# The second layer's activation: VectorE's clip and rest take the products from PSUM, not from ScalarE's copy

## The chip, the cores and the metric

One core of one Trainium2 chip (trn2). The metric is the device time of one execution of the whole program, in microseconds (us). The kernel before was run three times; one more execution was recorded by the hardware profiler.

## What is computed

Attention with a learned position bias, then two feed-forward layers, all in fp32 on 2304 tokens of 512 features:

```
x = attention(q, k, v, bias)                         # 4 x 8 heads, 576 x 64
x = max(max(x @ w1, x @ w2), x @ w3) @ w_out         # first layer, 768 hidden
h = x @ w_in                                         # second layer, 2304 x 2048
g = where(h >= 1, h, where(h <= -1, 0, (h + 1)**2 / 4))
out = g @ w_out                                      # 2304 x 512
```

The change is in the second layer. There the kernel uses that g is the square of 0.5 * clip(h, -1, 1) + 0.5, plus max(h - 1, 0), which the code calls clip (`tb`) and rest (`tc`).

## The kernel before

Weights, tokens and activations are each split into a high and a low fp32r part, and every product is three passes of TensorE (high times high, high times low, low times high).

The second layer runs last. Its work is ND = 72 items: 9 blocks of 256 tokens (b), with 8 items (j) in each, and n = 8b + j. An item holds two tiles of 128 hidden features, so 512 columns, one PSUM bank. For each n TensorE does in this order: `d_products(n)` (L1320), 24 matmuls into the item's bank; then `d_sums(n - 2)` (L1339), 21 matmuls that multiply the activation of the item two before with w_out. These are the seven products of a Strassen scheme, in seven banks. The seven sums run on over the 8 items of a block. `n_bank(n)` (L304) gives the bank of an item: 0, 1 and 2 for the first three, and bank 0 for all later ones, because banks 1 to 7 then hold the sums. So `d_products(n)` for n >= 3 waits until bank 0 has been read (L1324), and the very first `d_sums` waits until all of the first three banks have been read (L1348), since it writes banks 1 and 2.

The activation of item n goes back and forth between ScalarE and VectorE:

- ScalarE, L862: copies the bank (128x512) to `ta` in SBUF and counts `d_cp`. It waits for the products (`d_in`), and for the rest of the item before, as `ta` is single.
- VectorE, L1089: clip of `ta` into `tb`; L1090: rest of `ta` into `tc`. It waits for `d_cp` and for its own `g_lo` of the item before (`d_g_ok`).
- ScalarE, L866: square of `tb`, in place. VectorE, L1095: adds `tc`. VectorE, L1097 to L1102: four small sums for the Strassen scheme.
- ScalarE, L875 and L877: `g_hi`, in two parts. VectorE, L1104 and L1107: `g_lo`, in two parts, with `d_g_ok` at the end. `d_sums(n)` waits for that.

Each engine works through its own list in order, and some items have more in the list. In item j = 1 of every block but the first, behind the rest, `sums_first` of the block before (L844 on ScalarE, L1059 to L1064 on VectorE) takes sums from PSUM as TensorE ends them, and behind `g_lo` comes `sums_rest` (L849, L851; L1071 to L1077). Behind `g_lo` of j = 6, and in front of the clip of j = 7, VectorE does two each of `low_xd` (L1041), the low part of the next block's tokens; ScalarE does their high part (L831) in j = 5 and in front of j = 7. SyncE loads the weights of w_in in a ring of four; each load waits for `d_in` (L491).

Of the kernel before, what the change touches and what calls it, by code (L numbers as in the profile page):

```python
# [7 lines left out]
ALU = mybir.AluOpType  # L8
ACT = mybir.ActivationFunctionType
# [6 lines left out]
def build(nc, q, k, v, w1, b1, w2, moe_w1, moe_w2, moe_w3, moe_w_out, moe2_w_in, moe2_w_out, out):  # L16
# [55 lines left out]
    def sb(name, shape, dt=F32, c=None):  # L72
        return (c or ctx).enter_context(nc.sbuf_tensor(name, shape, dt))

    def sem(name):
        return ctx.enter_context(nc.semaphore(name))

    with ctx:
# [40 lines left out]
        with moe:  # L119
# [3 lines left out]
            ta = sb("ta", [P, 2 * SBT], c=moe)  # L123
            tb = sb("tb", [P, 2 * SBT], c=moe)
            tc = sb("tc", [P, 2 * SBT], c=moe)
# [17 lines left out]
        ps = ctx.enter_context(nc.psum_tensor("ps", [P, 8, 512], F32))  # L143
# [50 lines left out]
        win_in = [sem(f"win_in{r}") for r in range(WRING)]  # L194
        wt_in = [sem(f"wt_in{j}") for j in range(NPAIR)]
        d_x_hi, d_x_ok, d_x_used = sem("d_x_hi"), sem("d_x_ok"), sem("d_x_used")
        d_in, d_cp, d_clip, d_rest, d_sq, d_g = (sem(n) for n in
                                                 ("d_in", "d_cp", "d_clip", "d_rest", "d_sq", "d_g"))
        d_s13, d_s2, d_s4 = sem("d_s13"), sem("d_s2"), sem("d_s4")
        d_g_hi, d_g_ok = sem("d_g_hi"), sem("d_g_ok")  # L200
        d_item, d_acc, d_acc_cp, d_post = sem("d_item"), sem("d_acc"), sem("d_acc_cp"), sem("d_post")
# [89 lines left out]
        def ring_at(k):  # L291
            return k % WRING * WIN
# [8 lines left out]
        def x_slot(b, kt):  # L301
            return (KT * b + kt) % XRING

        def n_bank(n):  # L304

            return n if n < 3 else 0
# [355 lines left out]
        def _(act):  # L662
# [164 lines left out]
            def high_xd(b, kt):  # L827

                if b and kt >= XRING - KT:
                    act.wait_ge(d_x_used, (KT - 2) * (b - 1) + kt - 1)  # L830
                act.activation(xd_hi[:, x_slot(b, kt), :], xT[:, kt, x_cols(b)], ACT.Copy).then_inc(d_x_hi, 1)  # L831
# [7 lines left out]
            def sums_first(b):  # L839

                act.wait_ge(d_acc, 6 * b + 1)
                if b:
                    act.wait_ge(d_post, 7 * b)
                act.activation(u_sb, ps[:, P1_BANK, 0:HD], ACT.Copy).then_inc(d_acc_cp, 1)  # L844
# [9 lines left out]
            for n in range(ND):  # L854
                b, j = n // NPAIR, n % NPAIR
                if j == NPAIR - 1 and b + 1 < NSB:
                    high_xd(b + 1, 2)
                    high_xd(b + 1, 3)
                act.wait_ge(d_in, 2 * n + 2)
                if n:  # L860
                    act.wait_ge(d_rest, n)
                act.activation(ta[:, :], ps[:, n_bank(n), :], ACT.Copy).then_inc(d_cp, 1)  # L862
                if j == 1 and b:
                    sums_first(b - 1)
                act.wait_ge(d_clip, n + 1)
                act.activation(tb[:, :], tb[:, :], ACT.Square, scale=0.5, bias=0.5).then_inc(d_sq, 1)  # L866
                if j == 1 and b:
                    sums_rest(b - 1)
                if j == NPAIR - 3 and b + 1 < NSB:
                    high_xd(b + 1, 0)  # L870
                    high_xd(b + 1, 1)
                act.wait_ge(d_g, n + 1)
                if n >= 2:
                    act.wait_ge(d_item, n - 1)
                act.activation(g_hi[:, n % 2, 0:GA], tb[:, P:4 * P], ACT.Copy).then_inc(d_g_hi, 1)  # L875
                act.wait_ge(d_s4, n + 1)
                act.activation(g_hi[:, n % 2, GA:GS].rearrange("p (s c) -> p s c", s=4), s_sub,  # L877
                               ACT.Copy).then_inc(d_g_hi, 1)
# [4 lines left out]
        def _(dve):  # L883
# [197 lines left out]
            for n in range(ND):  # L1081
                b, j = n // NPAIR, n % NPAIR
                if j == NPAIR - 1 and b + 1 < NSB:
                    low_xd(b + 1, 2)
                    low_xd(b + 1, 3)
                dve.wait_ge(d_cp, n + 1)
                if n:
                    dve.wait_ge(d_g_ok, n)
                dve.tensor_scalar(tb[:, :], ta[:, :], -1.0, 1.0, ALU.max, ALU.min).then_inc(d_clip, 1)  # L1089
                dve.tensor_scalar(tc[:, :], ta[:, :], -1.0, 0.0, ALU.add, ALU.max).then_inc(d_rest, 1)  # L1090
                if j == 1 and b:
                    sums_first(b - 1)
                dve.wait_ge(d_rest, n + 1)
                dve.wait_ge(d_sq, n + 1)
                dve.tensor_tensor(tb[:, :], tb[:, :], tc[:, :], ALU.add).then_inc(d_g, 1)  # L1095
                dve.wait_ge(d_g, n + 1)
                dve.tensor_tensor(s1, a21, a22, ALU.add).then_inc(d_s13, 1)  # L1097
                dve.tensor_tensor(s3, a11, a21, ALU.subtract).then_inc(d_s13, 1)
                dve.wait_ge(d_s13, 2 * n + 2)
                dve.tensor_tensor(s2, s1, a11, ALU.subtract).then_inc(d_s2, 1)  # L1100
                dve.wait_ge(d_s2, n + 1)
                dve.tensor_tensor(s4, a12, s2, ALU.subtract).then_inc(d_s4, 1)  # L1102
                dve.wait_ge(d_g_hi, 2 * n + 1)
                dve.tensor_tensor(g_lo[:, n % 2, 0:GA], tb[:, P:4 * P], g_hi[:, n % 2, 0:GA].bitcast(F32), ALU.subtract)  # L1104
                dve.wait_ge(d_s4, n + 1)
                dve.wait_ge(d_g_hi, 2 * n + 2)
                dve.tensor_tensor(g_lo[:, n % 2, GA:GS].rearrange("p (s c) -> p s c", s=4), s_sub,  # L1107
                                  g_hi[:, n % 2, GA:GS].rearrange("p (s c) -> p s c", s=4).bitcast(F32),
                                  ALU.subtract).then_inc(d_g_ok, 1)
                if j == 1 and b:  # L1110
                    sums_rest(b - 1)
                if j == NPAIR - 2 and b + 1 < NSB:
                    low_xd(b + 1, 0)
                    low_xd(b + 1, 1)
# [4 lines left out]
        def _(pe):  # L1119
# [200 lines left out]
            def d_products(n):  # L1320

                b, j = n // NPAIR, n % NPAIR
                if n >= 3:
                    pe.wait_ge(d_cp, n)  # L1324
                for f in range(2):
                    k = 2 * n + f
                    pe.wait_ge(win_in[k % WRING], 16 * (k // WRING + 1))
                    for kt in range(KT):
                        if j == 0 and f == 0:
                            pe.wait_ge(d_x_ok, KT * b + kt + 1)  # L1330
                        at, s = ring_at(k) + kt * P, x_slot(b, kt)
                        for i, (lo, x) in enumerate(((0, xd_hi), (0, xd_lo), (KT * P, xd_hi))):
                            last = pe.matmul(ps[:, n_bank(n), f * SBT:(f + 1) * SBT], w_all[:, at + lo:at + lo + P],  # L1333
                                             x[:, s, :], start=(kt == 0 and i == 0), stop=(kt == KT - 1 and i == 2))
                        if j == NPAIR - 1 and f == 1 and kt < KT - 2:
                            last.then_inc(d_x_used, 1)
                    last.then_inc(d_in, 1)

            def d_sums(n):  # L1339

                b, j = n // NPAIR, n % NPAIR
                pe.wait_ge(d_g_ok, n + 1)
                if n == 0:
                    pe.wait_ge(c_y_ok, KT * NBLK)
                if b == 0:
                    pe.wait_ge(wt_in[j], 64 if j in PIECES else 16)
                if n == 0:
                    pe.wait_ge(d_cp, 3)  # L1348
                for i, (bank, g, w) in enumerate(PRODUCTS):
                    if j == 0 and b:  # L1350
                        if bank == P1_BANK:
                            pe.wait_ge(d_acc_cp, 3 * (b - 1) + 1)
                        elif i < 4:
                            pe.wait_ge(d_post, 7 * (b - 1) + i)
                        else:
                            pe.wait_ge(d_acc_cp, 3 * (b - 1) + min(i - 2, 3))
                    at = wt_at(j) + w * HD
                    for m, (x, lo) in enumerate(((g_hi, 0), (g_hi, TCOLS), (g_lo, 0))):
                        last = pe.matmul(ps[:, bank, 0:HD], x[:, n % 2, g * P:(g + 1) * P],  # L1359
                                         w_all[:, at + lo:at + lo + HD], start=(j == 0 and m == 0),  # L1360
                                         stop=(j == NPAIR - 1 and m == 2))
                    if j == NPAIR - 1 and i < 6:
                        last.then_inc(d_acc, 1)
                last.then_inc(d_item, 1)
# [31 lines left out]
```

## Time and profile before

| | us |
|---|---|
| median of 3 runs | 1020.13 |
| lowest and highest | 1017.62, 1020.18 |
| the profiled execution, its time | 1020.09 |
| its span in the trace | 1018.3 |
| TensorE busy | 991.1 (97% of the span) |
| VectorE busy | 616.4 (61%) |
| ScalarE busy | 509.4 (50%) |
| GpSimd busy | 347.4 (34%) |

The second layer starts at about 619 us of the span and goes to its end. Between the span and the time of the profiled execution lie 1.8 us that the trace does not show. In the trace PE is TensorE's matmuls, DVE is VectorE, ACT is ScalarE, and PEclk the clock that TensorE was granted, as a share of full speed. Matmuls overlap: one of 256 columns has a length of 0.28 us in the trace, and the next starts 0.12 us after it.

### The profile page before, as it was taken

Reading aid. Unit: us, or ns where it says so; the run is one execution under the profiler, and the core shown is the slowest. Engines: PE = TensorE matmul, PEld = TensorE weight load, DVE = VectorE, ACT = ScalarE, POOL = GpSimd, SP = SyncE. Lnnn points to the kernel's source line nnn. Section 1 sums busy time; section 2 is a strip of 40 time slices with the busy share of each in tenths; the row PEclk is TensorE's granted clock in tenths of the full one; section 3 lists DMA queues with packets and bytes.
Section 4 is the critical chain, followed back from the end, with each engine's and each line's share of the span. In section 5 each row is a group of like instructions: output and inputs, shape, how many; then the busy total and the mean of one; then the engine's idle time right before and its main releaser. Section 6 shows DMA issues by size and latency. Waiting matters only on the chain.

```text
span 1018.3 us, 23175 instructions
## 1 busy us (share of the span) xinstructions
PE 991.1 (97%) x8832; PEld 897.6 (88%) x8832; DVE 616.4 (61%) x1509; ACT 509.4 (50%) x1034; POOL 347.4 (34%) x522
## 2 busy tenths in 40 slices
PE   6979999999999999999999998999999999999998
PEld 3567777777767999999999998999999999999998
DVE  8957667666683242324231315677777877778776
ACT  8968778788793321212121213444554554545443
POOL 1059888888874878677300000000000000000000
PEclk9979999999999999999999999999999999999999
DMA  5982534425312464665510067866657667666772
GB/s 130 268 240 55 161 72 119 109 53 154 95 34 75 133 223 170 230 235 209 222 84 0 9 223 309 271 215 205 212 190 220 199 215 210 204 211 188 226 219 72
DMA packets 122149, 169.71 MB, mean 167 GB/s; under 512 B 67008, under 2 KB 84416, under 8 KB 120256
## 3 DMA queue, kind: packets, MB, share of 16 engines
q1 hardware_dynamic: 121952, 168.37, 53.0%
q8 instruction: 63, 1.03, 0.4%
q14 instruction: 38, 0.31, 0.1%
q10 hardware_dynamic: 96, 0.00, 0.0%
HBM read 129.64 MB, written 38.70 MB: 165 GB/s over the span
## 4 chain that ended last, share of the span: by engine, by line
PE 72%; DVE 2%; ACT 1%; issue 0%; DVEq 0%; ACTq 0%
PE ps L1265 22%; PE ps L1333 20%; PE ps L1359 18%; PE ps L1292 7%; PE ps L1216 2%; PE ps L1156 2%; PE ps L1177 1%; PE ps L1191 0%; DVE x_lo L979 0%; DVE tb L1095 0%; PE ps L1130 0%; ACT tb L866 0%; ACT ta L862 0%; DVE s_sb L926 0%; DVE g_lo L1107 0%
## 5 line engine op out<-in xcount | busy, mean ns | idle before, releaser
L1265 PE MATMUL ps<-x_hi,w_all 128*128 128x384 f32 x864 | 227.2, 336 | 3.0 <-DVE x_lo L979 1.8
L1333 PE MATMUL ps<-x_hi,w_all 128*128 128x256 f32 x1152 | 219.3, 283 | 1.2 <-DMA w_all<-win_scratch 1.2
L1359 PE MATMUL ps<-w_all,g_hi 128*128 128x256 f32 x1008 | 185.9, 284 | 2.6 <-ACT ta L862 2.4
L1333 PEld LDWEIGHTS ps<-x_hi,w_all 128*128 128x128 f32 x1152 | 184.8, 192 | 1.6 <-DMA w_all<-win_scratch 1.6
L1333 PE MATMUL ps<-x_lo,w_all 128*128 128x256 f32 x576 | 163.0, 283 | 0.0
L1265 PEld LDWEIGHTS ps<-x_hi,w_all 128*128 128x128 f32 x864 | 157.5, 189 | 5.3 <-DVE x_lo L979 2.3
L1359 PEld LDWEIGHTS ps<-w_all,g_hi 128*128 128x128 f32 x1008 | 158.3, 193 | 3.0 <-issue 2.6
L926 DVE CUSTOM_DVE_ANT_0 s_sb<-ps,bias_h 128x576 f32<-128x576 f32 (+1 forms) x160 | 114.8, 754 | 71.5 <-PE ps L1156 53.7
L1265 PE MATMUL ps<-x_lo,w_all 128*128 128x384 f32 x432 | 145.1, 336 | 0.0
L1359 PE MATMUL ps<-w_all,g_lo 128*128 128x256 f32 x504 | 143.1, 284 | 0.0
L586 POOL TENSOR_SCALAR probs<-probs,row_inv 128x576 f32<-128x576 f32 (+1 forms) x160 | 120.8, 766 | 18.7 <-DVE row_inv L956 18.1
L714 ACT ACTIVATE probs<-s_sb,row_min 128x576 f32<-128x576 f32 (+1 forms) x160 | 122.2, 769 | 1.8 <-DVE row_min L926 1.7
L1333 PEld LDWEIGHTS ps<-x_lo,w_all 128*128 128x128 f32 x576 | 110.6, 192 | 0.0
L1359 PEld LDWEIGHTS ps<-w_all,g_lo 128*128 128x128 f32 x504 | 97.4, 193 | 0.0
L1014 DVE TENSOR_TENSOR tb<-ps,ta 128x384 f32<-128x384 f32 x36 | 20.0, 557 | 121.9 <-PE ps L1265 121.3
L812 ACT ACTIVATE g_hi<-tc 128x384 fp32r<-128x384 f32 x36 | 18.9, 524 | 125.7 <-DVE tc L1021 125.7
L1265 PEld LDWEIGHTS ps<-x_lo,w_all 128*128 128x128 f32 x432 | 81.6, 189 | 0.0
L1292 PE MATMUL ps<-g_hi,w_all 128*128 128x384 f32 x288 | 78.7, 334 | 0.0
L1216 PE MATMUL ps<-p_t,v_in 128*64 128x320 f32 (+1 forms) x512 | 76.0, 418 | 0.0
L726 ACT ACTIVATE p_t<-ps 128x512 f32<-128x512 f32 x80 | 47.8, 597 | 49.3 <-PE ps L1177 48.4
L1156 PEld LDWEIGHTS ps<-qk_hi 64*128 64x128 f32 x320 | 36.7, 189 | 39.1 <-DVE row_min L926 22.6
L866 ACT ACTIVATE tb<-tb 128x512 f32<-128x512 f32 x72 | 45.6, 633 | 47.9 <-DVE tb L1089 47.9
(115 smaller groups left out, 1806.5 us busy)
## 6 DMA issues: line engine op xcount, KB each, us to landing
w_all<-win_scratch SPq DMA_DIRECT2D x144, 512.0 KB, 4.3
wt_scratch<-w_all SPq DMA_DIRECT2D x8, 1792.0 KB, 6.8
w_all<-wt_scratch SPq DMA_DIRECT2D x6, 1792.0 KB, 7.5
bias_scratch<-p_t SPq DMA_DIRECT2D x36, 296.0 KB, 4.6
win_scratch<-w_all SPq DMA_DIRECT2D x8, 1024.0 KB, 7.0
raw<-in_moe_w_out SPq DMA_DIRECT2D x22, 256.0 KB, 7.1
bias_h<-bias_scratch SPq DMA_DIRECT2D x16, 288.0 KB, 4.2
raw<-in_moe_w SPq DMA_DIRECT2D x18, 256.0 KB, 3.0
```

What stands on the lines that cost most here:

```text
L586: pool.tensor_scalar(pr, pr, row_inv[0:n, r, h:h + 1], 1.0, ALU.mult, ALU.mult).then_inc(p_norm, 1)
L714: act.activation(probs[0:n, r, h * S:(h + 1) * S], s_sb[0:n, (2 * u + h) % 4, :], ACT.Exp, scale=-1.0, bias=row_min[0:n, r, h:h + 1], accu ...
L726: act.activation(p_t[:, i % 2, :, :, t * P:t * P + HALF].rearrange("p h c j -> p (h c) j"), ps[:, X_BANK, :].rearrange("p (c j) -> p c j", ...
L866: act.activation(tb[:, :], tb[:, :], ACT.Square, scale=0.5, bias=0.5).then_inc(d_sq, 1)
L926: dve.tensor_tensor_reduce(s_sb[0:n, (2 * u + h) % 4, :].rearrange("p (c x) -> p c x", c=2), ps[0:n, 2 * h:2 * h + 2, 0:HC], bias_h[0:n, h ...
L1014: dve.tensor_tensor(tb[:, 0:BLK], ps[:, H_BANK_C[1], 0:BLK], ta[:, 0:BLK], ALU.max).then_inc(c_m1, 1)
L1156: return pe.matmul(ps[:, 2 * h + c, 0:HC], a[HALVES[h], i % 2, 0, t * P:(t + 1) * P], b[HALVES[h], i % 2, 1, c * HC:(c + 1) * HC], start=( ...
L1216: last = pe.matmul(ps[h * HALF:(h + 1) * HALF, O_BANK_A, 0:cols.stop - cols.start], v_in[:, i % 2, h, kt, :], tqk[:, i % 2, 0, cols] if kt ...
L1265: last = pe.matmul(ps[:, bank, 0:BLK], w[:, at:at + P], x[:, kt, :], start=(kt == 0 and n == 0), stop=(kt == KT - 1 and n == 2))
L1292: last = pe.matmul(ps[:, Y_BANK + dt, 0:BLK], w[:, at:at + P], g[:, ft % 2, :], start=(opens and i == 0), stop=(closes and i == 2))
L1333: last = pe.matmul(ps[:, n_bank(n), f * SBT:(f + 1) * SBT], w_all[:, at + lo:at + lo + P], x[:, s, :], start=(kt == 0 and i == 0), stop=(k ...
L1359: last = pe.matmul(ps[:, bank, 0:HD], x[:, n % 2, g * P:(g + 1) * P], w_all[:, at + lo:at + lo + HD], start=(j == 0 and m == 0), stop=(j = ...
```

## The change

```
@@ act, for n in range(ND)
-                act.wait_ge(d_in, 2 * n + 2)
-                if n:
-                    act.wait_ge(d_rest, n)
-                act.activation(ta[:, :], ps[:, n_bank(n), :], ACT.Copy).then_inc(d_cp, 1)
@@ dve, for n in range(ND)
-                dve.wait_ge(d_cp, n + 1)
+                dve.wait_ge(d_in, 2 * n + 2)
                 if n:
                     dve.wait_ge(d_g_ok, n)
-                dve.tensor_scalar(tb[:, :], ta[:, :], -1.0, 1.0, ALU.max, ALU.min).then_inc(d_clip, 1)
-                dve.tensor_scalar(tc[:, :], ta[:, :], -1.0, 0.0, ALU.add, ALU.max).then_inc(d_rest, 1)
+                dve.tensor_scalar(tb[:, :], ps[:, n_bank(n), :], -1.0, 1.0, ALU.max, ALU.min).then_inc(d_clip, 1)
+                dve.tensor_scalar(tc[:, :], ps[:, n_bank(n), :], -1.0, 0.0, ALU.add, ALU.max).then_inc(d_rest, 1)
@@ pe, d_products(n)
                 if n >= 3:
-                    pe.wait_ge(d_cp, n)
+                    pe.wait_ge(d_rest, n)
@@ pe, d_sums(n)
                 if n == 0:
-                    pe.wait_ge(d_cp, 3)
+                    pe.wait_ge(d_rest, 3)
```

The semaphore `d_cp` is gone. Nothing else changes; `ta` stays in use in the first layer.

## Rows read from the trace of the kernel before

**Rows 1.** The page's first part: busy us, share of span, instructions of each engine.

```profile
PE 991.1 (97%) x8832; PEld 897.6 (88%) x8832; DVE 616.4 (61%) x1509; ACT 509.4 (50%) x1034; POOL 347.4 (34%) x522
```

**Rows 2.** Busy time by stretch, 40 us of the second layer (stretch, length, engines, clock).

```profile
740.00:780.00 40.00, 40.00 (x335) 40.00 (x335) 30.36 (x77) 19.72 (x35) 0.00 (x0) 1.00 0.65 203
```

**Rows 3.** Timeline of an ordinary item (j = 5), PE, ACT and DVE (start, length).

```profile
735.73 0.28 PE L1333 MATMUL ps<-x_hi,w_all 128*128 128x256 f32 x1
...
738.37 0.28 PE L1333 MATMUL ps<-x_hi,w_all 128*128 128x256 f32 x1
...
736.05 0.60 ACT L862 ACTIVATE ta<-ps 128x512 f32<-128x512 f32 x1 [1.03 <-PE ps L1333]
737.14 0.63 ACT L866 ACTIVATE tb<-tb 128x512 f32<-128x512 f32 x1 [0.49 <-DVE tb L1089]
...
736.68 0.43 DVE L1089 TENSOR_SCALAR tb<-ta 128x512 f32<-128x512 f32 x1 [0.87 <-ACT ta L862]
737.03 0.42 DVE L1090 TENSOR_SCALAR tc<-ta 128x512 f32<-128x512 f32 x1
737.88 0.69 DVE L1095 TENSOR_TENSOR tb<-tb,tc 128x512 f32<-128x512 f32 x1 [0.43 <-ACT tb L866]
```

**Rows 4.** Groups of VectorE by line and form (count, busy us, mean ns, idle before).

```profile
L940 DVE COPY p_t<-ps 128x512 f32<-128x512 f32 x64 | 43.8, 684 | 2.3 <-PE ps L1177 2.3
...
L1089 DVE TENSOR_SCALAR tb<-ta 128x512 f32<-128x512 f32 x72 | 30.6, 425 | 37.7 <-ACT ta L862 36.6
...
L915 DVE TENSOR_SCALAR p_t<-ps,nconst 128x592 f32<-128x592 f32 x1 | 0.8, 833 | 4.6 <-DMA bias_scratch<-p_t 4.6
```

**Rows 5.** Timeline of items j = 1 and 2 of block 1, DVE and PE.

```profile
671.88 0.43 DVE L1089 TENSOR_SCALAR tb<-ta 128x512 f32<-128x512 f32 x1 [0.87 <-ACT ta L862]
...
672.56 0.42 DVE L1059 TENSOR_TENSOR raw<-ps,raw 128x256 f32<-128x256 f32 x1
...
678.33 0.42 DVE L1089 TENSOR_SCALAR tb<-ta 128x512 f32<-128x512 f32 x1
...
678.97 0.28 PE L1333 MATMUL ps<-x_hi,w_all 128*128 128x256 f32 x1
```

**Rows 6.** Timeline where the first products of the layer pass on, ACT, DVE, PE.

```profile
622.12 0.60 ACT L862 ACTIVATE ta<-ps 128x512 f32<-128x512 f32 x1 [2.08 <-PE ps L1333]
...
631.12 0.58 ACT L862 ACTIVATE ta<-ps 128x512 f32<-128x512 f32 x1
...
622.85 0.43 DVE L1089 TENSOR_SCALAR tb<-ta 128x512 f32<-128x512 f32 x1 [2.66 <-ACT ta L862]
...
627.49 0.43 DVE L1089 TENSOR_SCALAR tb<-ta 128x512 f32<-128x512 f32 x1
...
631.85 0.77 PE L1359 MATMUL ps<-w_all,g_hi 128*128 128x256 f32 x2 [2.40 <-ACT ta L862]
```

**Rows 7.** Busy time by stretch, as rows 2: idle times of TensorE and its clock.

```profile
58.00:61.40 3.40, 1.38 (x6) 1.05 (x8) 2.18 (x5) 2.16 (x4) 0.00 (x0) 0.51 0.98 281
61.40:64.80 3.40, 3.33 (x19) 2.41 (x19) 1.52 (x5) 1.74 (x7) 2.51 (x6) 0.50 1.00 339
...
624.60:628.05 3.45, 2.28 (x17) 1.87 (x16) 2.94 (x9) 1.74 (x4) 0.00 (x0) 1.00 1.01 370
...
631.46:634.87 3.41, 3.02 (x14) 3.05 (x15) 2.79 (x7) 0.87 (x2) 0.00 (x0) 0.50 0.89 360
```

**Rows 8.** Timeline of the last two `d_sums`, PE.

```profile
1010.53 0.40 PE L1359 MATMUL ps<-w_all,g_hi 128*128 128x256 f32 x2
1010.77 0.28 PE L1359 MATMUL ps<-w_all,g_lo 128*128 128x256 f32 x1
1011.27 0.50 PE L1359 MATMUL ps<-w_all,g_hi 128*128 128x256 f32 x2 [0.21 <-DVE g_lo L1107]
```

**Rows 9.** Timeline of VectorE from item j = 6 to j = 7 of block 2.

```profile
745.92 0.69 DVE L1107 TENSOR_TENSOR g_lo<-raw,g_hi 128x512 fp32r<-128x512 f32 x1 [0.30 <-ACT g_hi L877]
746.53 1.43 DVE L1041 TENSOR_TENSOR x_lo<-xT,x_hi 128x256 fp32r<-128x256 f32 x4
747.87 0.42 DVE L1089 TENSOR_SCALAR tb<-ta 128x512 f32<-128x512 f32 x1
```

More of the change, by code:

```diff
@@ L196, in build @@
         d_x_hi, d_x_ok, d_x_used = sem("d_x_hi"), sem("d_x_ok"), sem("d_x_used")
-        d_in, d_cp, d_clip, d_rest, d_sq, d_g = (sem(n) for n in
-                                                 ("d_in", "d_cp", "d_clip", "d_rest", "d_sq", "d_g"))
+        d_in, d_clip, d_rest, d_sq, d_g = (sem(n) for n in ("d_in", "d_clip", "d_rest", "d_sq", "d_g"))
         d_s13, d_s2, d_s4 = sem("d_s13"), sem("d_s2"), sem("d_s4")
```

## The prediction

> **What bounds the kernel now.** I read the busy shares first: TensorE is busy for 97% of the span [rows 1]. Then the second layer by stretch: TensorE is busy for 40 of 40 us at full clock, VectorE for 30.4, ScalarE for 19.7 [rows 2]. So nothing that shortens an activation can help in the steady state. The change can only open gaps on TensorE, or close the two it has in this layer: 2.40 us before the first `d_sums` [rows 6] and 0.21 us before the last [rows 8]. I therefore read the timeline for slack. The question is how long after the end of an item's products its bank is released, and when TensorE wants it back.
>
> The products of an item end at 735.73 + 0.28 = 736.01, and TensorE starts the next products at 738.37, 2.36 us later [rows 3]. Before, the bank was free 0.64 us after the products' end (0.04 to the start of the copy, 0.60 for it). TensorE goes from item to item in 5.40 us (45 matmuls at 0.12 us; 746.53 - 735.73 is two of them).
>
> **Part 1: the copy goes from ScalarE.** That frees 0.60 us per item on an engine that is half idle [rows 2, 3]: worth nothing by itself, since TensorE covers it. What it gives is an earlier clip: before, 0.67 us after the products' end (736.68), now 0.04, as ScalarE's copy had it. That is 0.63 us.
>
> **Part 2: clip and rest read PSUM.** From SBUF one takes 0.425 us. The trace before has no such instruction on 128x512 of PSUM. The low end is 0.425, as from SBUF. The high end is 0.83: L915, the one tensor_scalar from PSUM, which is 592 wide and has an operand from memory more. I take 0.69, from the copy of exactly this shape out of PSUM (684 ns, 64 times) [rows 4]. That is 0.26 more than now, for each of two instructions. Two VectorE instructions overlap by 0.08 us (clip to rest 0.35 for 0.43) [rows 3]. So the rest starts 0.60 after the clip starts and ends 0.60 + 0.69 = 1.29 after it (before: 0.77). The square waits for the clip alone, so everything behind it starts 0.26 later counted from the clip; the longer rest ends beside the square, and the add (before: 1.20 after the clip; now 1.46) still finds it done. An item's chain on VectorE, clip to next clip with no idle time for its input, was 627.49 - 622.85 = 4.64 us [rows 6]; it becomes 4.90. That is below 5.40, so VectorE keeps up in ordinary items, with 0.50 to spare, and an ordinary item's `g_lo` comes 0.63 - 0.26 = 0.37 earlier. Its bank is free at 0.04 + 1.29 = 1.33 after the products' end, before 2.36. Cost: nothing; cover: 1.03 us.
>
> A table of the Trainium skill (VectorE: DVE Perf Modes, the section on the TRN2 errata) charges an fp32 single-source operation 58 cycles plus half the elements from SBUF and 120 cycles plus all of them from PSUM. At its 0.96 GHz the growth would be an estimated 0.33 us and not 0.26, and with the terms below the sum would come out about 2.5 us higher. The trace's SBUF row (0.425 against the table's 0.33) does not bear the table out, so I stay with the rows. The same page's advice, to copy PSUM to SBUF first if many operations follow, speaks against this change.
>
> **Part 3: the bank's release moves from ScalarE's copy to VectorE's queue.** This costs. The rest now stands behind everything that VectorE still has to do for the item before, and behind it wait TensorE's next products, then all after them. Three places have more in the queue.
>
> (a) Item j = 2 of blocks 1 to 8, eight times. Before, its clip started at 678.33, late because VectorE did `sums_first` and `sums_rest` first; TensorE's next products started at 678.97 [rows 5], covered since ScalarE had copied already. Now: the clip of j = 1 starts at 671.88 - 0.63 = 671.25; L1059 follows two instructions of 0.60 spacing later, at 672.45 (before 672.56, 0.68 behind the clip). From L1059 to the next clip took 678.33 - 672.56 = 5.77 us, mostly VectorE's own work, which stays. So the clip of j = 2 starts at 678.22, its rest ends at 679.51, and TensorE resumes some 0.10 later, at 679.61, in place of 678.97: 0.64 us. After a wait its first two matmuls take 0.50 and not 0.40 [rows 8], 0.10 more. 8 x 0.74 = 5.9 us. The next clip, at 678.22 + 4.90 = 683.12, is back inside the cover, as TensorE itself is now 0.74 later.
>
> (b) Item j = 7 of blocks 0 to 7, behind four `low_xd`. The clip started at 747.87 [rows 9] and comes 0.37 earlier, 747.50; the rest ends at 748.79, and 0.10 on, at 748.89, TensorE can go. It wants to at 746.81 + 2.36 = 749.17. Cost: nothing, with only 0.28 us of cover.
>
> (c) The start. The first `d_sums` waited until ScalarE's third copy ended (631.12 + 0.58 = 631.70) and started at 631.85 [rows 6]. ScalarE's third copy did not need VectorE's item 1 complete; VectorE's third rest does. The first clip can start at 622.12, the third two chains later, at 622.12 + 2 x 4.90 = 631.92, and its rest ends at 633.21. With the same 0.15 TensorE goes at 633.36: 1.5 us later.
>
> The idle time there grows from 2.4 to 3.9 us, and it has an effect on the clock. After the 2.40 us TensorE ran at half clock from 631.46 to 634.87 [rows 7], of which 3.0 us fell on work; that lost about half of it. If the clock comes back at the same moment as before, only 1.5 us of work is slow (0.8 us gained); if a further such stretch follows, 4.9 us is (0.9 lost). The stretch from 58.00 is nearest, where TensorE also had little to do at half clock and the next one stayed at half [rows 7]. I take +0.8 and keep both ends.
>
> **Part 4: the end.** The last `d_sums` waited for `g_lo`, at 1011.27, when it could have gone at 1010.77 + 0.12 = 1010.89 [rows 8]. `g_lo` comes 0.37 earlier, at 1010.90. Gain: 0.4 us.
>
> The weight loads of SyncE wait for `d_in`, which TensorE still gives: they move only with TensorE. GpSimd has no part.
>
> **Sum.** +1.5 (start) + 0.8 (clock) + 5.9 (eight waits) - 0.4 (end) = +7.8 us on the profiled execution's 1020.09 (span 1018.3, 1.8 around it), which is 0.04 below the median: **1027.9 us**.
>
> **Rivals.**
>
> *PSUM reads cost VectorE no more than SBUF's: not slower.* Then the rest ends 0.77 after the clip. In (a) L1059 would have to wait for ScalarE's and TensorE's first sums, the next clip starts near 677.9, the bank is free at 678.7, before 678.97: no wait. At the start the third rest ends at 622.12 + 2 x 4.64 + 0.77 = 632.17, 0.5 late; the clock gives or takes 0.8; the end gives 0.4. Sum: 1020 (1019.4 to 1021.0). It decides at a clip and rest below about 0.53 us each, as 0.64 us of wait holds each excess four times. For it: ScalarE reads PSUM as fast as SBUF (0.60 for the copy, 0.63 for the square [rows 3]). Against: the copy's 684 ns [rows 4]. 7%.
>
> *The reads cost 0.83 each.* Growth 0.40: the start is 4 x 0.14 = 0.6 later, each wait of (a) takes 4 x 0.14 = 0.56 more (8 x = 4.5), and (b) loses its cover: clip 0.14 later, rest's end 0.42 later in all, 0.14 beyond the 0.28 and 0.10 for the restart, 8 x 0.24 = 1.9. The end's gain goes down to 0.3. Sum 7.8 + 0.6 + 4.5 + 1.9 + 0.1: 1035. 7%.
>
> *The clock falls at the eight waits.* If each brings a stretch at half clock of 3.4 us, 1.7 are lost each time: 1027.9 + 13.6 = 1041.5. Against: two idle times of about 0.6 us near 625 to 628 us, with TensorE busy for 2.28 of 3.45, and the clock stayed at 1.00 [rows 7]. 3%.
>
> *The change does not do what it says*: not likely, the diff names every wait and both operands; no chance of its own.
>
> **How the numbers follow.** The forecast has 83%. Its own range: 1.5 us less if the clock returns early, 1 less if restarts are free (0.10 x 8, and 0.05 in the wake), 1.5 more if the reads take 0.73, 1 more if the clock stays down longer; and an execution can lie 2.5 us below the profiled one, as one of the three runs does. That gives about 1023.5 to 1030.5. Towards the dearer reads I extend it to 1032; the rivals at 1020, 1035 and 1041.5 lie outside, 17%. 0.3% is 3.1 us, about what a measurement of this kernel can tell from no change. Slower by more: the forecast but for a twentieth of it (the waits half as long), and both dearer rivals, 0.89. Within 0.3%: that twentieth and most of the first rival, 0.09. Faster: the first rival with the clock's gain in runs as low as the lowest, 0.02.
>
> **What would show it.** Clip and rest at 0.69 us each; the rest's end the releaser of L1333 eight times, in total some 5 us; the wait before the first L1359 3.9 us, with the row of the clock at half behind it; the wait before the last gone; L1089 without idle time at j = 7, and no wait of TensorE there; ScalarE 43 us less busy (72 x 0.60). I am wrong if TensorE has no idle time at j = 2, or has some in ordinary items, or if the reads take another time than the copy.

## The result, and the profile after

The changed kernel took 1027.37 us (median of 10 runs, 1023.11 to 1030.73), the kernel before 1019.19 us in the same ten rounds (1017.39 to 1021.82). The medians are 8.2 us apart. The ratio of the two, taken over all their runs, is 1.0077, with a 95% interval of 1.006 to 1.0095: 7.8 us slower (6.1 to 9.7). The recorded execution of the changed kernel took 1026.83 us, with a span of 1025.0.

The page's first part, and then the same 40 us by stretch as in [rows 2]:

```profile
PE 992.3 (97%) x8832; PEld 897.5 (88%) x8832; DVE 654.2 (64%) x1509; ACT 467.7 (46%) x962; POOL 346.8 (34%) x522
```

```profile
740.00:780.00 40.00, 39.56 (x329) 39.36 (x329) 34.35 (x78) 15.59 (x29) 0.00 (x0) 1.00 0.70 208
```

ScalarE lost 41.7 us of work and VectorE got 37.8 us more. TensorE, which was busy for 40 of 40 us before, now has a small gap in that stretch. What it waited for in the second layer, by the view of waits (in total, times, longest):

```profile
PE ps L1354 <- DVE tc L1085: 4.1, 1, 4.1
PE ps L1328 <- DVE tc L1085: 3.5, 8, 0.4
PE ps L1328 <- DMA w_all<-win_scratch: 1.1, 2, 0.6
```

The lines have moved by five: L1328 is `d_products`, L1354 `d_sums`, L1084 the clip, L1085 the rest. The first wait is the start (2.40 before), the eight are new, the third was there before (2 times, 1.2 us in total). The wait before the last `d_sums`, 0.21 us in [rows 8], is gone. The groups of VectorE, to set against [rows 4]:

```profile
L1084 DVE TENSOR_SCALAR tb<-ps 128x512 f32<-128x512 f32 x72 | 49.7, 690 | 22.3 <-PE ps L1328 20.3
L1085 DVE TENSOR_SCALAR tc<-ps 128x512 f32<-128x512 f32 x72 | 49.1, 681 | 0.0
```

Both take what the copy of that shape out of PSUM takes (684 ns), not the 425 of the read from SBUF. The timeline of the changed kernel: the start (against [rows 6]), items j = 1 and 2 of block 1 (against [rows 5]), j = 6 and 7 of block 2 (against [rows 9]), and the last instruction on VectorE:

```profile
617.52 0.28 PE L1328 MATMUL ps<-x_hi,w_all 128*128 128x256 f32 x1
...
632.01 0.76 PE L1354 MATMUL ps<-w_all,g_hi 128*128 128x256 f32 x2 [4.07 <-DVE tc L1085]
...
640.16 0.40 PE L1354 MATMUL ps<-w_all,g_hi 128*128 128x256 f32 x2
...
620.69 0.69 DVE L1084 TENSOR_SCALAR tb<-ps 128x512 f32<-128x512 f32 x1 [1.95 <-PE ps L1328]
...
625.67 0.69 DVE L1084 TENSOR_SCALAR tb<-ps 128x512 f32<-128x512 f32 x1
...
630.57 0.69 DVE L1084 TENSOR_SCALAR tb<-ps 128x512 f32<-128x512 f32 x1
631.18 0.68 DVE L1085 TENSOR_SCALAR tc<-ps 128x512 f32<-128x512 f32 x1
...
672.76 0.69 DVE L1084 TENSOR_SCALAR tb<-ps 128x512 f32<-128x512 f32 x1 [0.45 <-PE ps L1328]
673.37 0.68 DVE L1085 TENSOR_SCALAR tc<-ps 128x512 f32<-128x512 f32 x1
673.96 0.41 DVE L1054 TENSOR_TENSOR raw<-ps,raw 128x256 f32<-128x256 f32 x1
...
679.74 0.68 DVE L1084 TENSOR_SCALAR tb<-ps 128x512 f32<-128x512 f32 x1
680.34 0.68 DVE L1085 TENSOR_SCALAR tc<-ps 128x512 f32<-128x512 f32 x1
...
680.36 0.28 PE L1354 MATMUL ps<-w_all,g_lo 128*128 128x256 f32 x1
681.08 0.39 PE L1328 MATMUL ps<-x_hi,w_all 128*128 128x256 f32 x1 [0.44 <-DVE tc L1085]
...
749.07 1.43 DVE L1036 TENSOR_TENSOR x_lo<-xT,x_hi 128x256 fp32r<-128x256 f32 x4
750.41 0.68 DVE L1084 TENSOR_SCALAR tb<-ps 128x512 f32<-128x512 f32 x1
751.01 0.68 DVE L1085 TENSOR_SCALAR tc<-ps 128x512 f32<-128x512 f32 x1
...
752.08 0.28 PE L1328 MATMUL ps<-x_hi,w_all 128*128 128x256 f32 x1
...
1021.79 0.42 DVE L1072 TENSOR_TENSOR raw<-raw,acc_sb 128x256 f32<-128x256 f32 x1
```

How to read the eight waits: the rest of j = 2 ends at 680.34 + 0.68 = 681.02, and TensorE's products start at 681.08. With no wait they would have started at 680.36 + 0.12 = 680.48. That is 0.60 us, and 0.1 more for the restart. The record calls only 0.44 of it idle, since the last matmul is drawn 0.28 long. So a wait of x in the record costs x + 0.26.

The whole second layer can be cut into three parts by such rows: first products to first `d_sums`; from there to the second `d_sums`, in which the slow matmuls lie; and from there to the end of VectorE's last instruction. For the kernel before the rows are these, with 631.85 of [rows 6]:

```profile
618.97 0.28 PE L1333 MATMUL ps<-x_hi,w_all 128*128 128x256 f32 x1
...
638.65 0.40 PE L1359 MATMUL ps<-w_all,g_hi 128*128 128x256 f32 x2
...
1015.04 0.42 DVE L1077 TENSOR_TENSOR raw<-raw,acc_sb 128x256 f32<-128x256 f32 x1
```

Worked out so for every record but those with a moved wait, whose first `d_sums` is cut in two (us):

| kernel | to first sums | to second sums | the rest | layer |
|---|---|---|---|---|
| before | 12.88 | 6.80 | 376.81 | 396.49 |
| changed | 14.49 | 8.15 | 382.05 | 404.69 |
| start as before | 12.87 | 6.96 | 381.98 | 401.81 |
| changed at the start only | 14.48 | 6.95 | 376.80 | 398.23 |
| changed, late sums | 14.48 | 6.73 | 376.45 | 397.66 |
| release moved, no PSUM read | 14.05 | 6.95 | 378.97 | 399.97 |
| both mends | 12.89 | 6.95 | 376.45 | 396.29 |
| changed, two small reads more | 15.32 | 6.95 | 392.04 | 414.31 |
| changed, again a | 14.48 | 6.96 | 381.98 | 403.42 |
| changed, again b | 14.47 | 7.95 | 381.96 | 404.38 |
| changed, again c | 14.48 | 6.96 | 381.96 | 403.40 |

The layer of the changed kernel is 8.20 us longer: 1.61 at the start, 1.35 in slow matmuls, 5.24 in the rest (eight times 0.70, less 0.36 at the end). What comes before the layer was 1.45 us shorter in this record; it has no part in the change and differs from record to record. The first and third parts repeat within 0.1 us; so they tell kernels apart that the whole time, which scatters by 2 or 3 us, hardly does.

### The profile page after: what moved, and what is told of

It reads as the page before. It is cut to its first block, busy times and chain, and to the rows that moved or that the text cites. A ratio compares the mean times of both kernels' runs of the same rounds, so it can differ in the third digit from the quotient of the medians.

```text
span 1025.0 us, 23032 instructions
## 1 busy us (share of the span) xinstructions
PE 992.3 (97%) x8832; PEld 897.5 (88%) x8832; DVE 654.2 (64%) x1509; ACT 467.7 (46%) x962; POOL 346.8 (34%) x522
## 4 chain that ended last, share of the span: by engine, by line
PE 66%; DVE 6%; issue 2%; ACT 1%; DVEq 0%; ACTq 0%
PE ps L1260 22%; PE ps L1328 18%; PE ps L1354 14%; PE ps L1287 7%; PE ps L1211 2%; PE ps L1151 2%; DVE tb L1084 1%; PE ps L1172 1%; DVE tb L1090 1%; ACT g_hi L872 1%; DVE tc L1085 1%; PE ps L1186 0%; DVE raw L1072 0%; DVE raw L1066 0%; DVE raw L1054 0%
## 5 line engine op out<-in xcount | busy, mean ns | idle before, releaser
L1328 PE MATMUL ps<-x_hi,w_all 128*128 128x256 f32 x1152 | 220.7, 284 | 4.7 <-DVE tc L1085 3.5
L1328 PEld LDWEIGHTS ps<-x_hi,w_all 128*128 128x128 f32 x1152 | 185.4, 192 | 6.7 <-DVE tc L1085 5.2
L1354 PE MATMUL ps<-w_all,g_hi 128*128 128x256 f32 x1008 | 186.5, 285 | 4.1 <-DVE tc L1085 4.1
L1328 PE MATMUL ps<-x_lo,w_all 128*128 128x256 f32 x576 | 163.2, 283 | 0.0
L1354 PEld LDWEIGHTS ps<-w_all,g_hi 128*128 128x128 f32 x1008 | 158.8, 194 | 4.3 <-issue 4.2
L1354 PE MATMUL ps<-w_all,g_lo 128*128 128x256 f32 x504 | 143.5, 285 | 0.0
L585 POOL TENSOR_SCALAR probs<-probs,row_inv 128x576 f32<-128x576 f32 (+1 forms) x160 | 120.3, 762 | 20.1 <-DVE row_inv L951 19.5
L1328 PEld LDWEIGHTS ps<-x_lo,w_all 128*128 128x128 f32 x576 | 110.9, 193 | 0.0
L1354 PEld LDWEIGHTS ps<-w_all,g_lo 128*128 128x128 f32 x504 | 97.7, 194 | 0.0
```

The lines of the kernel that those rows point to most:

```text
L585: pool.tensor_scalar(pr, pr, row_inv[0:n, r, h:h + 1], 1.0, ALU.mult, ALU.mult).then_inc(p_norm, 1)
```

## The experiments

Every difference below is a ratio to the kernel before, run on the same chip in the same rounds, less 1 and times 1019 us. The ratio goes by all runs, so it can lie some tenths of a us beside the difference of the medians.

**Is it the start, or the eight waits?** The first kernel undoes the change for items 0 to 2; the second makes it there alone.

```
# start as before: items 0 to 2 the old way
+                if n < 3:
+                    act.wait_ge(d_in, 2 * n + 2)
+                    if n:
+                        act.wait_ge(d_rest, n)
+                    act.activation(ta[:, :], ps[:, n_bank(n), :], ACT.Copy).then_inc(d_cp, 1)
...
+                src = ta[:, :] if n < 3 else ps[:, n_bank(n), :]
...
-                if n >= 3:                   # d_products
+                if n == 3:
+                    pe.wait_ge(d_cp, 3)
+                elif n > 3:
                     pe.wait_ge(d_rest, n)
...
-                    pe.wait_ge(d_rest, 3)    # d_sums(0)
+                    pe.wait_ge(d_cp, 3)
# changed at the start only: the kernel before, with
-                dve.wait_ge(d_cp, n + 1)     # for n < 3: wait_ge(d_in, 2 * n + 2)
+                src = ta[:, :] if n >= 3 else ps[:, n_bank(n), :]
...
```

> The changed kernel, but items 0 to 2 go the old way (ScalarE's copy, the bank released by it); from item 3 on clip and rest read PSUM. Theory (the bank's release stands in VectorE's queue: one longer wait at the start with slow matmuls behind it, and eight waits at item j = 2): the start is as before, 2.40 us idle and one stretch at half clock, the eight waits stay at 0.44 us of idle in the record, 0.7 with the restart. Time: 5 to 5.5 us over the kernel before, 2.5 to 3 under the changed one. Rival (the start and the clock carry nearly all of it, the eight waits are made up elsewhere): within 1 us of the kernel before.

> The kernel before, but items 0 to 2 go the new way: the change in 3 of its 72 items. Theory: the wait before the first sums is about 4.0 us in place of 2.4, with about 6.8 us at half clock behind it in place of 3.4; no other wait. Time: 2.5 to 3 us over the kernel before. Rival (PSUM reads cost in every item): three items of 72 cost next to nothing, under 0.5 us.

The start as before: ratio 1.0053 (1.0038 to 1.0068), 5.4 us over the kernel before. Changed at the start only: 1.0041 (1.0028 to 1.0055), 4.2 us. The waits of TensorE in the second layer, of the first and then of the second:

```profile
PE ps L1339 <- DVE tc L1094: 3.5, 8, 0.4
PE ps L1365 <- ACT ta L862: 2.2, 1, 2.2
```

```profile
PE ps L1365 <- DVE tc L1094: 3.6, 1, 3.6
PE ps L1339 <- DMA w_all<-win_scratch: 1.6, 2, 0.9
PE ps L1365 <- DVE g_lo L1111: 0.2, 1, 0.2
```

The two effects come apart in the records: with the start as before the third part is 5.17 us longer than in the kernel before, and the first is not; with the change at the start only the first is 1.60 longer, and the third is not. The second is 0.15 longer in both. The rival of each falls. What was expected of the clock in the second did not come: its record shows one short stretch at half clock, so by its record the start costs 1.7 us. By its runs it costs 4.2, more than the 2.5 to 3 expected, and even the low end of the interval (2.9 to 5.6) is above 1.7. The section on the clock below comes back to this. The eight waits are the larger part in either case.

**Is it the read, or who releases the bank?** One kernel keeps all of VectorE's reads from PSUM and takes work out of the queue in front of the clip of j = 2. The other keeps the copy and the reads from SBUF and only lets TensorE wait for the rest.

```
# changed, late sums: the last two lines of sums_rest are sums_last
-                if j == 1 and b:
-                    sums_rest(b - 1)         # behind g_lo
...
+                if j == 2 and b:
+                    sums_rest(b - 1)         # behind the rest
+                if j == 3 and b:
+                    sums_last(b - 1)
# release moved: the kernel before, with
-                    pe.wait_ge(d_cp, n)
+                    pe.wait_ge(d_rest, n)
-                    pe.wait_ge(d_cp, 3)
+                    pe.wait_ge(d_rest, 3)
```

> The changed kernel, but the four instructions of sums_rest no longer stand in front of the clip of item j = 2: two come behind the rest of j = 2, two behind the rest of j = 3. Clip and rest read PSUM in all items. Theory: TensorE has no wait on the rest at j = 2; the start stays as in the changed kernel. Time: 5.5 to 6 us under the changed one, 2 to 3 over the kernel before. Rival (the reads themselves, or VectorE's larger load, hold TensorE up): the same time as the changed one, within 1 us, with the waits at another item.

> The kernel before with its copy and its reads from SBUF, but TensorE waits for the rest and not for the copy: the release moved, no read from PSUM by VectorE. Theory: the release costs by itself: third rest done 1.2 us after the third copy at the start, slow matmuls behind it for up to 1.3 us, and eight waits at j = 2 of 0.2 us and 0.1 for the restart each. Time: 3.5 to 5 us over the kernel before. Rival (only the dearer reads cost): within 0.5 us of the kernel before.

Late sums: 1.002 (1.0008 to 1.0032), 2.0 us over the kernel before, as expected. Its start is that of the kernel changed at the start only, which took 4.2; the two intervals overlap. Release moved: 1.0055 (1.004 to 1.007), 5.6 us, over the 3.5 to 5 expected, which the interval (4.1 to 7.1) reaches; its record has 3.48 us, the low end of what was expected and, as with the start alone, less than its runs show. Their waits of TensorE:

```profile
PE ps L1361 <- DVE tc L1089: 3.8, 1, 3.8
PE ps L1335 <- DMA w_all<-win_scratch: 1.4, 2, 0.7
```

```profile
PE ps L1359 <- DVE tc L1090: 3.3, 1, 3.3
PE ps L1333 <- DMA w_all<-win_scratch: 1.5, 2, 0.8
PE ps L1359 <- DVE g_lo L1107: 0.2, 1, 0.2
```

With four instructions of VectorE moved behind the rest all eight waits are gone, though every read is as dear as in the changed kernel; the third part is even 0.36 us under the kernel before, the gain at the end. So in this part dear reads and a fuller VectorE cost nothing by themselves. And with no dear read at all the release in VectorE's queue costs: 1.17 us at the start and 2.16 in the rest, 0.27 a wait (expected 0.3). At those eight places the view of waits shows no idle time of the matmuls, as the drawn length of the last one hides the gap; the weight loads have it:

```profile
  DMA w_all<-win_scratch: 3.4, 4
  DVE tc L1090: 1.7, 8
```

(these are two lines of the answer on `d_products`, L1333: what its instructions, loads and matmuls, sat idle for). The dearer reads bring the wait at j = 2 from 0.27 to 0.70. Both rivals fall: of the 5.6 us of the waits 2.2 are the release's alone, the rest needs both.

**Both mends together.** Items 0 to 2 as in the first kernel, the sums as in the third.

> The changed kernel with both mends: items 0 to 2 the old way, and sums_rest behind the rest of j = 2 and j = 3. Clip and rest read PSUM in 69 of 72 items. Theory (VectorE's dearer reads cost only where they delay the bank's release): no wait is left that the kernel before does not have, and the one before the last sums is gone. Time: that of the kernel before less 0.4 us, so not to be told from it. Rival (the reads cost by themselves, as VectorE is busy for most of the time): 2 us or more over the kernel before.

0.9996 (0.9985 to 1.0008): the time of the kernel before, with clip and rest from PSUM in 69 of 72 items. The rival falls. The third part, 376.45 against 376.81, has the expected 0.36; in the whole time it can't be told from nothing.

**How large was the cover at j = 7?** The prediction left it at 0.28 us. In the changed kernel the rest of j = 7 ends at 751.01 + 0.68 = 751.69 and TensorE goes on at 752.08, 0.39 later. After the rest of j = 2 TensorE goes on 0.06 later (681.08 less 681.02), so 0.33 of this is cover. Two small reads more in each item take more than that. Their results are not used.

```
+                for i in range(2):
+                    dve.tensor_scalar(ta[:, i * P:(i + 1) * P], ps[:, n_bank(n), i * P:(i + 1) * P],
+                                      -1.0, 0.0, ALU.add, ALU.max)
                 dve.tensor_scalar(tc[:, :], ps[:, n_bank(n), :], -1.0, 0.0, ALU.add, ALU.max).then_inc(d_rest, 1)
```

> The changed kernel with two more small reads of the bank (128x128, results unused) in front of the rest, in every item: the rest ends 0.42 us later, and what is behind it on VectorE 0.3. Theory: each wait at j = 2 grows by 0.84 (idle about 1.3 us in the record); at j = 7 the 0.28 us of cover that the changed kernel had left is used up and a wait of some 0.44 us with 0.1 for the restart appears, eight times; the start is 1.0 later. Ordinary items stay covered. Time: 12 us over the changed kernel (11 to 14). Rival (there was more cover than that, or the delay adds up in every item): no wait at j = 7 and 8 us, or waits in all 72 items and 25 us or more.

Ratio 1.0191 (1.0177 to 1.0204), 19.5 us over the kernel before and so 11.6 over the changed one (1.0191 less 1.0077). The waits of TensorE in its second layer, and from its timeline the waits at j = 7 and j = 2:

```profile
PE ps L1330 <- DVE tc L1087: 11.2, 16, 1.2
PE ps L1356 <- DVE tc L1087: 4.7, 1, 4.7
```

```profile
665.90 0.39 PE L1330 MATMUL ps<-x_hi,w_all 128*128 128x256 f32 x1 [0.17 <-DVE tc L1087]
...
683.60 0.39 PE L1330 MATMUL ps<-x_hi,w_all 128*128 128x256 f32 x1 [1.24 <-DVE tc L1087]
```

Sixteen waits: eight at j = 2, grown by 0.80 (1.24 for 0.44), and eight at j = 7 of 0.17 + 0.26 = 0.43 (expected 0.54). The wait is smaller than expected since the rest of j = 7 ends only 0.66 later than in the changed kernel, and not 0.72: 2.63 us after the end of the item's products, against 1.97. Less the 0.33 of cover that is 0.33, and with the 0.1 of the restart 0.43. Eight times 0.80 + 0.43 is 9.8 us; the third part grew by 10.0. No other item has a wait. The start became 0.84 us longer (expected 1.0). So the cover at j = 7 is real and about as small as was read off.

**Does the start need to wait at all?** The first `d_sums` writes banks 1 and 2 only in its sixth and seventh product, but waits for them before its first. In three kernels that wait moves: the one with both mends, the changed one, and the one before.

```
-                if n == 0:
-                    pe.wait_ge(d_cp, 3)      # d_rest in the changed kernel
                 for i, (bank, g, w) in enumerate(PRODUCTS):
+                    if n == 0 and i == 5:
+                        pe.wait_ge(d_cp, 3)
```

> As e5_both, and the wait of the first sums for the reading of banks 1 and 2 stands in front of the sixth product, the first that writes one of them, and not in front of all seven. Theory: fifteen matmuls (1.8 us) fill most of the 2.4 us of idle time, some 0.5 us of it stay, and if TensorE's clock then stays at full speed another 1.3 to 1.6 us come back. Time: 3 to 3.6 us under the kernel before. Rival (the clock falls as before): 1.8 to 2.3 us under it.

> The changed kernel with that wait moved in front of the sixth product alone. Theory: the idle time at the start goes from 4.07 us to about 2.2, in the midst of the first sums, and the clock is at half for 3.4 us at most. Time: 2 to 3.5 us under the changed kernel, so 5 to 6 over the kernel before: the eight waits of j = 2 (0.70 each, less the 0.36 at the end) stay.

> The kernel before with the wait of the first sums moved in front of their sixth product, nothing else. If the gain of the run with both mends and the moved wait is the moved wait's, this one gains as much but for the 0.4 us at the end: 2 to 3 us under the kernel before, idle time about 0.4 us. If the reads from PSUM are needed for the gain, it is within 1 us of the kernel before.

| kernel with the wait moved | ratio to the kernel before | idle at the wait |
|---|---|---|
| both mends | 0.997 (0.9958 to 0.9982) | 0.4 |
| changed | 1.0045 (1.0031 to 1.006) | 2.4 |
| before | 0.9979 (0.9968 to 0.999) | 0.2 |

The waits of the first and of the second, then the matmul behind the wait in the first:

```profile
PE ps L1372 <- ACT ta L862: 0.4, 1, 0.4
```

```profile
PE ps L1328 <- DVE tc L1085: 3.5, 8, 0.4
PE ps L1354 <- DVE tc L1085: 2.4, 1, 2.4
```

```profile
631.13 0.51 PE L1372 MATMUL ps<-w_all,g_hi 128*128 128x256 f32 x2 [0.40 <-ACT ta L862]
```

With both mends it is 3.1 us under the kernel before by the ratio and 2.5 by the medians (1016.43 against 1018.89): expected 3 to 3.6. The times alone do not exclude the rival with the fallen clock (1.8 to 2.3), as the interval is 1.8 to 4.3; the record does, with the granted clock at full speed all through the first sums. In the kernel before the same edit brings 2.1 (expected 2 to 3). The intervals overlap, so nothing says that the reads from PSUM add to it; the version with both mends and the moved wait is the fastest that was run only by that margin. In the records the layer takes 393.2 us with both mends and 393.3 in the kernel before with the same edit, against 396.5. In the changed kernel the edit takes off about 3.3 us (1.0077 less 1.0045; expected 2 to 3.5) and leaves 4.6 over the kernel before, a little less than the 5 to 6 expected, inside the interval. The eight waits are untouched.

**How long is the clock down?** The first record of the changed kernel has TensorE at half clock for two stretches on end, the kernel with the change at the start only has one, behind 3.6 us of idle time against 4.1. So the changed kernel was recorded three times more.

> The changed kernel once more, for one more recorded execution: how long TensorE is at half clock behind the idle time of about 4 us. It was 6.8 us in the first record. If the length goes with the idle time alone, it is 6.8 again; if it also hangs on where in time the idle falls, it is 3.4 in some executions and 6.8 in others, and the start costs 1.6 us plus 0.1 to 1.4.

> As the run before it: a third record of the changed kernel, with the same two readings (6.8 us at half clock each time, or 3.4 in some).

> As the two runs before it: a fourth record of the changed kernel, with the same two readings (6.8 us at half clock each time, or 3.4 in some).

Granted clock by stretch (the column behind POOL's), in the first record and in the next one:

```profile
631.00:634.40 3.40, 2.39 (x11) 2.42 (x12) 2.62 (x7) 0.63 (x1) 0.00 (x0) 0.54 0.65 258
634.40:637.80 3.40, 3.40 (x18) 3.40 (x17) 0.32 (x1) 0.88 (x2) 0.00 (x0) 0.50 0.00 0
637.80:641.20 3.40, 3.40 (x29) 3.40 (x29) 1.77 (x4) 0.28 (x2) 0.00 (x0) 0.95 0.39 77
```

```profile
631.00:634.40 3.40, 3.14 (x17) 3.17 (x18) 1.88 (x6) 0.18 (x1) 0.00 (x0) 0.62 0.54 200
634.40:637.80 3.40, 3.40 (x27) 3.40 (x27) 1.25 (x2) 1.05 (x2) 0.00 (x0) 0.88 0.00 0
637.80:641.20 3.40, 3.40 (x30) 3.40 (x30) 2.54 (x6) 0.83 (x2) 0.00 (x0) 1.00 0.74 218
```

In two of the four records the half clock lasts long, 6.8 us (second part 8.15 and 7.95), in two short, 3.4 us (6.96 each), with the same kernel. The second reading holds: the slow matmuls cost 0.15 us more than before, or 1.15 to 1.35, and the kernel's code does not set which.

What the long ones have in common is when the clock fell. The share of a stretch tells the moment: 0.54 over 3.40 us is 0.3 us at full speed and the rest at half, so it fell at 631.3 in the first record, 0.7 us before TensorE went on (632.01); 0.62 is 0.8 us at full speed, so it fell at 631.8 in the second, 0.5 us after TensorE went on. For the third record, the other long one, the stretch and where TensorE goes on in it; then the latter for the second:

```profile
631.00:634.40 3.40, 2.46 (x11) 2.50 (x12) 2.56 (x7) 0.63 (x1) 0.00 (x0) 0.50 0.68 266
631.93 0.77 PE L1354 MATMUL ps<-w_all,g_hi 128*128 128x256 f32 x2 [3.94 <-DVE tc L1085]
```

```profile
631.26 0.47 PE L1354 MATMUL ps<-w_all,g_hi 128*128 128x256 f32 x2 [3.46 <-DVE tc L1085]
```

In the third it had fallen before 631.00, over 0.9 us before TensorE went on; in the fourth, short like the second, it fell 0.3 after. In every other record with a half clock there it fell at the latest 1.4 us after and at the earliest 0.5 us before TensorE went on (0.4 in the kernel before, 0.5 with late sums), and it lasted 3.4 us, even behind the longest idle time of all, 4.73 us with two small reads more. Why it falls earlier or later is not shown.

Four records are few, but the record has the mean granted clock of every run. In the four kernels with more than 3 us of idle time at the start it is lower than that of the kernel before in the same rounds, by 0.0020 (late sums) to 0.0026 (release moved); over 1019 us that is 2.0 to 2.6 us of clock. In those with 2.4 us or less it is within 0.0006. With the change at the start only it is 0.9909 against 0.9930, some 2.1 us. Part of this can lie on idle time, where it costs nothing, so it is an estimate from above: the start costs up to about 1.6 + 2.1 = 3.7 us. That is inside the interval of this kernel's runs, where the 1.7 of its one record is not: that record seems to be of one of the cheaper executions.

## Why the prediction was right

The forecast was 7.8 us, to 1027.9; measured were 1027.4, 8.2 us over the kernel before by the medians and 7.8 by the ratio. The mechanism was right in its main part, the eight waits and the start. That the whole agrees to some tenths is luck, as the interval is 1.8 us to either side and the term for the clock was right only as a mean. Step by step:

- **What bounds.** TensorE did, and what moved the time was gaps on it. Right; ScalarE's relief by itself was worth nothing.
- **The price of a read** was taken from the copy of the same shape, 0.69 us; clip and rest take 0.690 and 0.681. The rival of cheap reads (0.425) and that of dear ones (0.83) fell on this row. They grew by 0.265 and 0.261.
  By the table of the Trainium skill (VectorE: DVE Perf Modes, the section on the TRN2 errata) the growth would be an estimated 0.33 us; the runs do not bear that out.
- **The chain** of an item was to grow to 4.90 us; 630.57 - 625.67 is 4.90. Ordinary items have no wait.
- **(a) The eight waits** were put at 0.74 each and measure 0.70, 5.6 us for 5.9. The releaser, the item and the number are as forecast; the 0.04 is the hand-over, forecast at 0.10 and measured at 0.06. The kernel with late sums shows the cause: take VectorE's own work from in front of the clip, and they go. The size also needs the dearer reads, by which a wait of 0.27 becomes one of 0.70.
- **(b) j = 7**: no wait, with 0.33 us of cover for a forecast 0.28 (0.29 with the hand-over at 0.10, as forecast). That it was so near is shown by the kernel with two small reads more.
- **(c) The start** was put at 1.5 and measures 1.61. The difference is mostly in the first item's chain: from the first to the second clip are 4.98 us and not 4.90.
- **The clock** was put at +0.8, between -0.8 and +0.9. Four records show +0.15 twice, +1.15 and +1.35: 0.7 in the mean; the mean clocks of the runs of the start-only kernel allow up to about 2. The value was right as a mean and is no value of any one execution. The picture behind it did not hold: it let the clock fall at the same moment as before, with 1.5 or 4.9 us of work at half clock; the moment moves from execution to execution, and 3.4 us of work were slow in the short records and 5.7 and 6.1 in the long ones. The low end, a gain, did not occur in these four; with late sums, which has the same start, it was a gain of 0.07.
- **Part 4, the end**: 0.4 forecast, 0.36 measured.
- **The signs.** The eight waits were to show some 5 us in total and show 3.5: the forecast of the sign left out that the last matmul is drawn 0.28 long, which hides 0.16 of each wait. ScalarE was to have 43 us less work and has 41.7 less.
- **The rival of a clock that falls at the eight waits** fell: behind 0.44 us of idle time, and in the kernel with two small reads more behind 1.24, the granted clock stayed at full speed.

The steps sum to 1.61 + 0.7 + 5.6 - 0.36 = 7.6 us; the runs show 7.8 with an interval from 6.1 to 9.7. The single kernels were measured with intervals of some 1.2 to 1.5 us to either side, and the start alone (4.2) and the waits alone (5.4) sum to more than the whole; only the records, not the times, tell such parts apart.

## What to carry to other kernels

A copy out of PSUM that looks needless may be what releases the bank. Before it is taken away, ask which engine's queue the release moves to, what that engine still has in front of it in its worst item, and compare this with the time until TensorE wants the bank back: here the bank is read 1.3 us after the products' end in an ordinary item, against 2.36, but in one item of eight only 2.90 after it (681.02, with TensorE due at 680.48). Where such a wait appears, work that nobody is waiting for can be put behind the read. And a wait belongs in front of the instruction that needs it: moving one from the first to the sixth product took 2.1 us off the kernel before.

## What was not expected of the hardware

TensorE's clock after an idle time depends on more than the idle time. The same kernel, with 3.5 to 4.1 us idle at the same place, came back to full speed after 3.4 us in two records and after 6.8 us in two. The late ones are those in which the clock had fallen longest (0.7 us and more) before TensorE went on. An idle time of 2.2 to 2.4 us was enough to bring it to half clock in all records that have one there (before, start as before, both mends, and the changed kernel with the wait moved), and so was one of 1.8 us in the first layer of the kernel before (half clock from 467.6 on). With 0.2 and 0.4 us (the two other kernels with the wait moved) it stayed at full speed, and so it did behind the eight times 1.24 us.
